# Attention and two MLP layers on one Trainium2 core: low parts shared between GpSimd and VectorE, the first weight combination in smaller pieces, and the kept weight sums later in the step

## The reference: what is computed

```python
# attention: 4 batches, 8 heads, 576 positions, head size 64, causal, window 128, linear bias
scores = scale * np.matmul(q, k.transpose(0, 1, 3, 2))
scores = np.where(mask, scores + bias[None], -1000000000.0)
attn = np.exp(scores - np.max(scores, axis=-1, keepdims=True))
attn = attn / (np.sum(attn, axis=-1, keepdims=True) + 1e-09)
x = (attn @ v)                       # as 2304 tokens x 512
# first MLP, 512 -> 2048 -> 512
h = np.maximum(x @ w_in, 0.0)
x = h * h @ w_out
# second MLP, same sizes
h = x @ w_in2
g = h * np.cos(h)
return g @ w_out2
```

## Time and profile before

| | us |
|---|---|
| median of 3 runs | 883.9 |
| lowest and highest | 879.07, 887.78 |
| the profiled execution | 886.29 |
| its span, first to last instruction | 884.5 |
| PE busy | 856.3 |
| DVE busy | 647.9 |
| ACT busy | 523.7 |
| POOL busy | 88.1 |
| mean granted clock of TensorE | 0.992 of full speed |

### The profile page before, as it was taken

How to read it: one execution, slowest core, us unless ns; L and a number is a source line. 1 busy time by engine, 2 the same in 40 slices (tenths; PEclk the granted TensorE clock), 3 DMA queues, 4 the chain that set the end, 5 groups by cost and what they waited for, 6 DMA issues and landing times.

```text
span 884.5 us, 16152 instructions
## 1 busy us (share of the span) xinstructions
PE 856.3 (97%) x5840; PEld 773.4 (87%) x5840; DVE 647.9 (73%) x1443; ACT 523.7 (59%) x1143; POOL 88.1 (10%) x186
## 2 busy tenths in 40 slices
PE   7998789999999999999999999999999999999997
PEld 5887679999998999989999988988889888888886
DVE  6889688886766857767767687777787777767664
ACT  7888443433343433243343588777787877877774
POOL 6689700000000000000000000000000000000000
PEclk9999999999999999999999999999999999999999
DMA  5787226456578687768777755555575555565522
GB/s 194 250 252 267 70 108 230 161 216 231 183 260 293 230 310 289 261 225 301 254 262 263 234 189 161 186 191 191 167 253 186 187 196 189 192 225 190 194 72 72
DMA packets 72047, 185.34 MB, mean 210 GB/s; under 512 B 7200, under 2 KB 19488, under 8 KB 69920
## 3 DMA queue, kind: packets, MB, share of 16 engines
q1 hardware_dynamic: 71104, 183.23, 60.5%
q10 hardware_dynamic: 864, 1.08, 0.3%
HBM read 141.82 MB, written 42.47 MB: 208 GB/s over the span
## 4 chain that ended last, share of the span: by engine, by line
PE 88%; DVE 4%; DMA 2%; ACT 2%; issue 2%; POOL 1%; SPq 0%; DVEq 0%
PE psum L717 37%; PE psum L751 21%; PE psum L756 14%; PE psum L758 7%; PE psum L660 3%; PE psum L572 2%; PE psum L618 2%; DMA k_raw<-k_t 1%; DMA wout<-kept_out_lo 1%; DVE hidden_sum L1209 1%; POOL probs L495 1%; DVE g_lo L1263 1%; PE psum L581 1%; DVE probs L1089 0%; DVE work L1258 0%
## 5 line engine op out<-in xcount | busy, mean ns | idle before, releaser
L717 PE MATMUL psum<-xt_hi,comb 128*128 128x384 f32 x1344 | 399.1, 339 | 7.5 <-DVE part_b L1209 4.4
L717 PEld LDWEIGHTS psum<-xt_hi,comb 128*128 128x128 f32 x1344 | 249.5, 189 | 24.0 <-issue 9.9
L751 PE MATMUL psum<-wout,g_hi 128*128 128x512 f32 x576 | 180.2, 394 | 0.3 <-DVE g_lo L1263 0.3
L930 ACT ACTIVATE g_hi<-work 128x384 fp32r<-128x384 f32 x192 | 97.2, 517 | 96.2 <-DVE work L1258 56.0
L756 PE MATMUL psum<-g_hi,wout 128*128 128x512 f32 x384 | 150.4, 395 | 0.0
L1263 DVE TENSOR_TENSOR g_lo<-work,g_hi 128x384 fp32r<-128x384 f32 x192 | 102.2, 552 | 44.2 <-ACT g_hi L930 42.9
L717 PE MATMUL psum<-x_lo,comb 128*128 128x384 f32 x384 | 129.3, 337 | 0.0
L751 PEld LDWEIGHTS psum<-wout,g_hi 128*128 128x128 f32 x576 | 105.9, 188 | 12.4 <-issue 0.7
L751 PE MATMUL psum<-wout,g_lo 128*128 128x512 f32 x288 | 113.9, 395 | 0.0
L758 PE MATMUL psum<-g_hi,wout 128*128 128x256 f32 x384 | 108.3, 282 | 0.0
L717 PE MATMUL psum<-xt_lo,comb 128*128 128x384 f32 x288 | 97.9, 340 | 0.0
(11 more groups left out here) (101 smaller groups left out, 1295.4 us busy)
## 6 DMA issues: line engine op xcount, KB each, us to landing
comb<-comb SPq DMA_DIRECT2D x80, 768.0 KB, 4.9
wout<-wout SPq DMA_DIRECT2D x48, 512.0 KB, 4.8
comb<-comb SPq DMA_DIRECT2D x8, 1792.0 KB, 7.0
comb<-kept SPq DMA_DIRECT2D x8, 1792.0 KB, 7.5
wout_raw<-w_out SPq DMA_DIRECT2D x48, 256.0 KB, 4.4
comb<-comb SPq DMA_DIRECT2D x40, 256.0 KB, 3.2
v_raw<-v SPq DMA_DIRECT2D x16, 512.0 KB, 3.4
raw<-w_in SPq DMA_DIRECT2D x32, 256.0 KB, 7.0
```

The costliest lines, as they stand in the source:

```text
L717: last = pe.matmul(psum[:, H_BANK + i % 2, 0:NH], wi, mi[:, k, :], start=first, stop=True, skip_group_check=True)
L751: last = pe.matmul(psum[:, Y_BANK + c, :], g[:, r, tok], w, start=start and m == 0, stop=True, skip_group_check=True)
L930: act.activation(g_hi[:, r, cols], work[i][:], ACT.Copy).then_inc(g_hi_ready, 1)
```

## The change

1. The first combined weights are loaded and made two slots earlier and in smaller pieces: `LATE_LOADS` goes from 4 to 2, the sums stand in slots 4 and 5, the high parts in 6 and 7, the low parts in slots 8 to 11 (`first_lo`: 512, 256 and 256, 512 and 256 columns).
2. POOL makes only three of the seven low activation parts: B11 in slot 15, T3 and T2 in slot 16. DVE makes B21 in slot 16, T1 and T4 in slot 17 and B22 in slot 18. Before B21 DVE waits until POOL has done its three, because the semaphore counts in one order.
3. The sums of the activations stand before `invert_sums` in slots 11 to 14, not after `copy_x`.
4. `SPLIT_ORDER` is split into `HI_ORDER` and `LO_ORDER`, and `HI_AT`, `LO_AT` and `FIRST_HI` follow, also for the later blocks.
5. In the even steps from 8 to 22 `kept_weight_sums` stands right before part_c, `kept_weights_lo` where the low part of the sums stood, and `kept_sums_lo` after the last sum of the step.

```diff
-LATE_LOADS = 4
+LATE_LOADS = 2
 FIRST_T = 11
-POOL_WEIGHTS = 6
-FIRST_HI = {12: ["B11"], 13: ["T3"], 14: ["T2"], 15: ["T1"], 16: ["B21", "T4"], 17: ["B22"]}
+FIRST_HI = {11: ["B11"], 12: ["T3"], 13: ["B21"], 14: ["T2"], 15: ["B22"], 16: ["T1", "T4"]}
+FIRST_LO = {15: ["B11"], 16: ["T3", "T2"]}
...
-SPLIT_ORDER = ["B11", "T3", "T2", "T1", "B21", "T4", "B22"]
+HI_ORDER = ["B11", "T3", "B21", "T2", "B22", "T1", "T4"]
+LO_ORDER = ["B11", "T3", "T2", "B21", "T1", "T4", "B22"]
 T_AT = ["T3", "T1", "T2", "T4", None, None, None, None]
-HI_AT = [[], ["B11"], ["T3"], ["T2"], ["T1", "B21"], ["T4"], ["B22"], []]
-LO_AT = [None, None, "B11", "T3", "T2", "T1", "B21", "T4"]
+HI_AT = [[], ["B11"], ["T3", "B21"], ["T2"], ["B22"], ["T1"], ["T4"], []]
+LO_AT = [None, None, "B11", "T3", "T2", "B21", "T1", "T4"]
...
-                if LATE_LOADS <= p < LATE_LOADS + 2:
-                    load_raw(p - LATE_LOADS)
-                elif LATE_LOADS + 2 <= p < LATE_LOADS + 2 + W_RING:
-                    load_wout(p - LATE_LOADS - 2)
-                elif p == LATE_LOADS + 8:
+                if p == LATE_LOADS:
+                    load_raw(0)
+                elif p == LATE_LOADS + 3:
+                    load_raw(1)
+                elif LATE_LOADS + 4 <= p < LATE_LOADS + 4 + W_RING:
+                    load_wout(p - LATE_LOADS - 4)
+                elif p == FIRST_T + 1:
                     save_comb(0)
                     load_raw(2)
...
-            def first_weights_lo():
...
-            def first_sums_lo(a):
...
+            def first_lo(a, b):
+
+                pool.wait_ge(comb_hi_ready, 1 if b <= 3 else 2)
+                source = raw[:, 0, a + 1:b + 1, :] if b <= 3 else sums[:, a - 3:b - 3, :]
+                last = pool.tensor_tensor(comb[:, 0, 1, a:b, :], source, comb[:, 0, 0, a:b, :].bitcast(F32), ALU.subtract)
+                if b in (3, 7):
                     last.then_inc(comb_ready, 1)
...
             def split_moving(t, name):
-                order = SPLIT_ORDER.index(name)
-                dve.wait_ge(xt_hi_ready, len(MOVING) * t + order + 1)
+                if t == 0 and name == "B21":
+                    dve.wait_ge(xt_ready, LO_ORDER.index(name))
+                dve.wait_ge(xt_hi_ready, len(MOVING) * t + HI_ORDER.index(name) + 1)
...
             def first_step(n):
                 t, j = divmod(n, STEPS)
                 job, turn = job_of(n), j == 1
-                if job is not None and n % 2 == 0:
-                    kept_weight_sums(job)
                 part_b_sum(n)
                 lo_g(n - 1, 2)
...
-                if job is not None and n % 2 == 0:
-                    kept_weights_lo(job)
                 lo_g(n - 1, 3)
                 split_wout(2 * n - 2)
                 if not makes_weights(n):
                     split_at(n)
+                if job is not None and n % 2 == 0:
+                    kept_weight_sums(job)
                 part_c_sum(n)
...
                 if job is not None and n % 2 == 0:
-                    kept_sums_lo(job)
+                    kept_weights_lo(job)
...
                 c12_sum(n)
                 make_g(n, 3)
+                if job is not None and n % 2 == 0:
+                    kept_sums_lo(job)
...
+                if FIRST_T <= s < FIRST_T + 4:
+                    moving_sum(0, T_AT[s - FIRST_T])
                 if 1 <= s < PAIRS + 1:
                     invert_sums(s - 1)
...
-                if FIRST_T <= s < FIRST_T + 4:
-                    moving_sum(0, ["T3", "T1", "T2", "T4"][s - FIRST_T])
                 if s == PAIRS:
+                    split_moving(0, "B21")
                     weight_sums(1)
                 elif s == PAIRS + 1:
+                    split_moving(0, "T1")
+                    split_moving(0, "T4")
                     weights_lo(1)
                 elif s == PAIRS + 2:
+                    split_moving(0, "B22")
                     sums_lo(1)
```

More of the change, by code:

```diff
@@ L517, in first_sums_hi, with first_moving_lo @@
                     .then_inc(comb_hi_ready, 1)
[L519 to L528 removed]
+            def first_lo(a, b):
[3 more added lines that the diff above has]
+                if b in (3, 7):
                     last.then_inc(comb_ready, 1)
[L531 to L532 removed]
+            def first_moving_lo(name):
                 pool.wait_ge(t_done, T_READ[name])
[L534 removed]
+                pool.wait_ge(xt_hi_ready, HI_ORDER.index(name) + 1)
                 pool.tensor_tensor(moving_lo(0, name), moving_raw(0, name), moving_hi(0, name).bitcast(F32),
```

41 lines of the change are left out of this document (16 added, 25 removed).

## The result

| | before | after |
|---|---|---|
| median of 20 runs each | 884.25 us | 881.58 us |
| lowest and highest | 879.07 to 888.15 | 880.14 to 883.54 |
| profiled execution | 886.29 us | 881.39 us |
| its span, mean granted clock | 884.5 us, 0.992 | 879.6 us, 0.994 |

The changed kernel takes 0.9969 of the time of before, 95% interval 0.9957 to 0.9982: 2.7 us less, where 6.1 less were forecast (877.8 us). The two profiled executions differ by 4.9 us, since that of before was 2.0 above its median. The runs of before also spread over 9.1 us, those of after over 3.4 us.

What follows compares the result with a forecast made beforehand. PE was taken as the bound, busy 856.3 of 884.5 us. 886.3 - 6.5 + 2.9 - 2.5 = 880.2 us against the profiled execution; with the median 2.4 us below it, 877.8 us, range 870.5 to 884.5.

Steps and rivals of the forecast that it cites:

- part 5: Even steps 8 to 22: moving the kept sums ends two part_b waits; -6.5 us, bounds -7.8 and -1.4.
- transition, up to step 1: Slots 16 to 18: DVE's B21 waits for POOL's T2, and DVE has more splits; +2.9 us, bounds +0.7 and +4.6.
- slow clock behind the start of step 1: Stretch 120 to 130 at clock 0.83: its 1.7 us going was only in the transition's lower bound, +0.7.
- attention: Attention slots: bias waits go, -1.1 us, and the wait for k goes, -1.4; -2.5 us, between 0 and -3.2.
- -2 x 3.9 + 1.3: Steps 10 and 18 each save 2.21 us wait and 1.7 slow clock; steps 8, 10, 16, 18 lose 0.3 to 0.4.
- The margin of 0.3 us: Even steps: part_c ends at 9.1 after product 0, PE wants it for product 5 at 9.4.
- Both bounds: Transition: +0.7 if one slow stretch goes and POOL is sooner, +4.6 if a further slow stretch comes.
- k is there about when PE asks: Wait for k at 88.20: SP issues the store some 3 us earlier, so the 1.43 us wait goes; -1.4 us.
- the transition loses its slow clock: Rival: one or two slow stretches of 1.7 us don't come, job steps lose nothing; about 874 us, chance 0.22.
- the attention gains nothing: Rival: k still late; 880.3 us, or 882.0 with a dearer transition; chance 0.20 for no gain or dearer transition.
- the waits return at j = 2: Rival: the store lands later than 7.1, the wait returns before part_c, one 3.9 us stays; 881.7 us, chance 0.06.
- The slower one: Rival: DVE bounds the job steps, PE waits for part_c and the last sum, 12.8 us; 889.3 us, chance 0.07.

Runs made afterwards that it cites:

- the five with the old first step: Profiles: the unchanged kernel three times, the changed kernel without part 5 (ratio 1.0026), and the unchanged kernel plus only parts 1 and 3 (one run, 886.1 us).
- the four with the old attention and transition: Profiles: the unchanged kernel three times, and the unchanged kernel plus only part 5 (881.17 us, ratio 0.9964).
- the four with the new: Profiles: the changed kernel twice, it without part 5 (ratio 1.0026), and it with kept sums late only in steps 10 and 18 (ratio 0.9951).
- five profiles of the old order: Profiles: the unchanged kernel three times, it plus only part 5 (ratio 0.9964), and it plus only parts 1 and 3 (one run, 886.1 us).

## Why the prediction was wrong

The direction and the range (870.5 to 884.5) held; the size did not, -2.7 us against -6.1. By its own steps, with the means over the profiles (part 5: the five with the old first step against after; the others: the four with the old attention and transition against the four with the new):

| term | predicted | profiles | timed |
|---|---|---|---|
| part 5 | -6.5 | -4.1 | -3.2 alone, -5.0 on top of parts 1 to 4 |
| transition, up to step 1 | +2.9 | +3.0 | |
| slow clock behind the start of step 1 | | -0.8 | |
| attention | -2.5 | -1.8 | |
| parts 1 to 4 together | +0.4 | +0.4 | +2.3 (0.4 to 4.2) alone, +0.5 on top of part 5 |
| sum | -6.1 | -3.7 | -2.7 (-3.8 to -1.6) |

Part 5 holds 2.4 of the 3.4 us that are missing. The attention gave 0.7 less than forecast, and the slow clock behind the start of step 1, which the forecast had only as a bound, made up for it. The other 1.0 lies between the few profiles and the timed runs, and no step can be named for it.

**Part 5, the step that failed.** It was "-2 x 3.9 + 1.3": what the two waits cost, less what the moved sums cost. Both numbers were too kind. The waits cost 2 x 3.4 us in four profiles of five, and the moved sums 3.0.

The 3.9 took the 1.7 us of slow clock behind a wait as part of its price, for both waits. Of five profiles, the one that it was read from is the only one in which step 10 had that slow clock; it loses 8.0 us in the two steps. In the other four the two steps lose 2.8 and 4.0 us above the free 15.65, 6.8 and not 7.8. The 16 steps from 8 to 23 take 258.4 us in the first profile and 257.2, 257.2, 257.1 and 257.2 in the others. Against after's 253.4 that is 5.1 us in the one and 3.8 in the four, 4.1 in the mean. The extra 1.2 us is also part of why the profiled execution stood above its median: the forecast took that excess off the level, and counted it in the saving as well.

The 1.3 should have been 3.0 (4 steps of 0.62 and 4 of 0.13). DVE in step 8 of after:

```profile
235.68 0.56 DVE L1263 TENSOR_TENSOR g_lo<-work,g_hi 128x384 fp32r<-128x384 f32 x1 [1.92 <-ACT g_hi L929]
...
236.75 0.95 DVE L1139 TENSOR_TENSOR x_lo<-x,xt_hi 128x768 fp32r<-128x768 f32 x1
237.62 0.42 DVE L1153 TENSOR_TENSOR sums<-raw 128x256 f32<-128x256 f32 x1
...
239.09 0.55 DVE L1209 TENSOR_TENSOR part_c<-psum,part_a 128x384 f32<-128x384 f32 x1
...
244.82 0.55 DVE L1209 TENSOR_TENSOR hidden_sum<-psum,part_b 128x384 f32<-128x384 f32 x1
```

and PE in the same step (the last row of the three is product 0 of step 9):

```profile
239.79 0.42 PE L716 MATMUL psum<-xt_hi,comb 128*128 128x384 f32 x1
...
245.00 0.28 PE L757 MATMUL psum<-g_hi,wout 128*128 128x256 f32 x1
245.52 0.41 PE L716 MATMUL psum<-xt_hi,comb 128*128 128x384 f32 x1 [0.24 <-DVE hidden_sum L1209]
```

Counted from ACT's 230.57, `lo_g` starts at 5.11, the split of `wout` at 5.58, `split_at` at 6.18, the sums at 7.05, and part_c ends at 239.64, which is 9.07: the forecast had 5.11, 5.6, 6.2, 7.1 and 9.1. The last sum ends at 245.37, 14.8, forecast 15.0. The chain on DVE was right to 0.2 us. The deadlines were not. DVE's times count from the start of ACT's copy, and PE's units of 1.04 us were counted from the same moment. But PE starts the piece behind product 0 at 230.37, 0.20 us ahead of ACT's copy. So it was ready for product 5 at 239.65 + 0.12 = 239.77 (its pieces of this shape follow each other by 0.12 us), 9.2 behind ACT's start and not 9.4, and the hand-over from DVE takes 0.15 (239.64 to 239.79). The margin of 0.3 us was none. In a step without a wait, product 0 of the next step starts 14.4 behind ACT's copy (steps 9 and 11), and not 14.6. And a late operand costs more than the idle time that the profile shows: at product 5 the profile shows no wait, but its first matmul takes 0.42 us in place of 0.34 and the next starts 0.25 behind it in place of 0.17, and each of the eight steps is 0.13 us longer for it. At 245.52 it shows 0.24 us, while PE was ready at 245.00 + 0.12 = 245.12: 0.40 late, and 0.08 more in the first matmul. So the last sum costs 0.48 us in the four steps with j = 0 and 2, 1.9 us where 1.3 were counted, and part_c 0.13 in all eight, 1.0 us where nothing was counted.

**The transition** was right in its mean up to step 1, +3.0 for +2.9, in part by luck. Against the profile of before its chain is right: from `scores(15)` to `values(14)` it is 18.4 us after and 16.8 before, +1.6 for the predicted +1.7; to `values(15)` 27.7 and 25.8, +1.9 for +2.0. But before's own transition is a draw between 31.9 and 36.2 us. Against the mean of the four old ones it is +1.1 to `values(14)` and +1.5 to `values(15)`, and the way from there to step 1 takes 7.9 us in all four old ones and 8.8 to 9.8 in the new, +1.5 where B22 was priced at +0.9. Both bounds came true in part: a further slow stretch came ahead of step 1 (0.66 and 0.83 in after), and that behind the start of step 1 went in three profiles of four.

**The attention** gave 1.8 us for 2.5: `scores(15)` starts at 88.20, 88.53, 88.47 and 87.10 with the old slots and at 86.14, 87.14, 85.46 and 86.34 with the new. The biases' waits went as forecast (-1.1), the moved sums take 0.95 us as forecast, POOL was out of their way. "k is there about when PE asks" was half right: SP issues the load at 78.09 and not 80.73:

```profile
74.73 0.58 SPq L350 DMA_DIRECT2D comb<-comb  x1
...
78.09 1.24 SPq L338 DMA_DIRECT2D k_raw<-k_t  x1
```

It lands 2 us earlier, but PE asks earlier as well and waits for most of a microsecond. With the store behind the load the last slot is 1.2 us shorter still, and from `scores(11)` to `scores(15)` it is 22.5 us where the four old profiles have 25.2 in the mean: the term for k was the one that fell short, and the whole -2.5 was there to be had.

**The rivals.** That the transition loses its slow clock fell: over 100 to 130 it is 5.1 us in after and was 3.4. That the attention gains nothing fell, with k late in part. That the waits return at j = 2 fell: no wait for part_b is left. The slower one was right in its place, product 5 and the last sum, and wrong in its size, 3.0 us in eight steps where it would have needed over 7. It was priced from a wait of a microsecond a step, and its small version was the one that mattered.

## What to carry to other kernels

Before a wait is priced, look at it in more than one execution: the idle time repeats, what follows it (a stretch of slow clock, a stretched instruction beside POOL) may not, and a gain read from the one profile that has it is too large. Where a chain is moved up against a deadline, count both from one instruction's start in the trace, add the hand-over, and take a margin under about 0.3 us as none, times the number of steps. And when work is shared out between two engines ahead of something that a third waits for, look at the order at that point before who does it: here the new sharing cost time, and the copy that PE needs put first, with the low parts behind, gave the largest gain.

## What was not expected of the hardware

- A two-input VectorE sum of 0.41 us was held for 5.72, 5.71 and 5.94 us in three of five profiles of the old order, across three POOL instructions in a row, and for about 2 us in the other two. Three of the five are of one unchanged kernel and gave 2.03, 1.91 and 5.71. What decides between the outcomes is open.
- Two waits of PE of the same 2.2 us, at places ahead of which PE was busy without a gap for 15 us in all five, are followed by the lower clock level in one of five profiles and in five of five.
- A wait so short that the profile shows no idle time cost 0.13 us, and one shown as 0.24 us cost 0.48: the first matmul behind it is longer by 0.08 us, and the last one before it counts as busy for 0.28 us where the next normally starts after 0.12.
